# Attention written out step by step, with two score buffers, one bank for turned rows and routing counts, 112-wide two-head tiles, and a shorter last chunk

## The chip, the cores and the metric

The kernel runs on one core of one Trainium2 chip. The metric is device time in microseconds (us) of one launch. Shares of the time are read in one profiled execution. TensorE is PE in the profile (PEld is its weight load), VectorE is DVE, ScalarE is ACT, GpSimd is POOL, and SP is the engine that only issues transfers.

## The reference

A gated linear attention (batch 4, 8 heads, 768 tokens, head size 48) feeds a top-1 mixture of 8 experts, and that feeds a normed gated MLP over 3072 tokens of width 384:

```python
for t in range(S):                       # attention
    state = f[:, :, t, :, None] * state + einsum('bhd,bhe->bhde', k[:, :, t], v[:, :, t])
    y[:, :, t] = einsum('bhd,bhde->bhe', q[:, :, t], state)
logits = x @ w_gate + modality_bias[modality_id]          # experts, x = the 3072 rows of y
e_idx = argmax(logits, axis=1)
h = maximum(x[mask] @ w1[e], 0.0); out[mask] = gate_w[mask, None] * (h @ w2[e])
xn = x / rms * rms_g                                      # MLP
out = (silu(xn @ w_gate) * (xn @ w_val)) @ w_out
```

## The kernel before, in words

The program has two large parts. `attention` takes the first 158 us, `experts` (the experts, then the MLP) the rest. Between them stands a fallback, `general_attention`, which is skipped when a flag is zero; entering and leaving these parts is a barrier of all engines.

In `attention` the 24 tiles of 128 tokens (number n = 4c + b, chunk c = 0 to 5 of the sequence, batch entry b = 0 to 3) pass through a software pipeline. A function `steps` calls one `step(c, b, ...)` for each tile number plus four more (c = 6, called CH), and each engine has its own `step`. `tile(c, b, back)` names the tile that a part of the step works on: the one `back` places behind. The order on each engine is simply the order in which its step is written, and semaphores (`masked`, `x_kept`, `yT_kept` ...) join the engines. Heads go in pairs: one of the two in rows 0 to 47, the other in rows 64 to 111 of the 128 partitions (PAD = 64).

In the step of tile m PE does, in this order: the key turn of tile m-1 (transposes into `ks_ps`, L730), the scores of m-1 (`sc_ps`, L738), the turn-and-gate product of m-3 (`x_ps`, L749, 96 output columns and 8 routing logits per head pair), the state's growth of m-2 (`ds_ps`, L720), and the output of m-2 (`yT_ps`: from the old state L766, from the scores L773). DVE does: scaled keys and queries kT, qT of tile m (L617, L618), the running sum of m+1 (L605), the mask of the scores of m-1 (L627), `grown` of m-2 (L635), and the logits of m-3 read from `x_ps` (L646). ACT does the exponentials, copies `ks`, fades the state (L556), copies `x_group` (L567) and `yT` (L575). POOL clamps the gates of later tiles (L496) and scatters finished rows to the experts' regions in HBM (L137).

Once per chunk the routing is done: `choose` on DVE at b = 2 (L100 to L113), `count` on PE at the end of b = 3 (two small matmuls into `rt_ps`, L117, L118), `place` on DVE at the next b = 0 (L126 to L133). In chunks 3 and 5 a `pick` follows on DVE (L197 to L205): it chooses the expert whose weights SP loads ahead (L208 to L218). In the last four steps ACT and DVE also split these weights into a high and a low part (`hi_w1`, `lo_w1`, L222, L226), and PE turns the first rows of that expert (L233), which SP loads (L218) after the scatters of chunk 3 have landed. The last four scatters stand on POOL behind `place` of chunk 4, and POOL waits for their landing before it leaves the part.

The loop over chunks 2 to 5 is a loop in hardware with two chunks in its body; `ahead` wraps some operations in a branch.

Of the kernel before, what the change touches and what calls it, by code (L numbers as in the profile page):

```python
# [19 lines left out]
PAD = 64  # L20
PR = H // 2
# [223 lines left out]
def attention(nc, qkf, v, w_gate, modality, bias, ident, rt, first, w1, w2, decay, flag, x_regions):  # L245
# [9 lines left out]
    with ExitStack() as ctx:  # L255
# [41 lines left out]
        rt_ps = ps("rt_ps", [P, 3, E])  # L297
        flag_ps = rt_ps[:, 2, 0:1]
# [40 lines left out]
        xT_ps = sc_ps[:].rearrange("p a j t -> p (a j t)")[:, 0:KD * TM].rearrange("p (k t) -> p k t", k=KD)  # L339

        def steps(eng, step):

            for i in range(2 * B):
                step(i // B, i % B, i // B, nullcontext)
            with eng.Fori(1, CH // 2) as i:
                for half in range(2):
                    for b in range(B):  # L350
                        step(i * 2 + half, b, half, (lambda: eng.If(i < CH // 2 - 1)) if half else nullcontext)
            for b in range(B):
                step(CH, b, 0, None)
# [10 lines left out]
        def ahead(b, steps_ahead, more):  # L364
            return more() if b + steps_ahead >= B else nullcontext()

        RT_MADE = 7
        BIAS_STEPS = 4
        PICKS = CH // 2 - 1
# [3 lines left out]

        def x_pairs(s):
            return x_ps[:, s % 2, 0:PR * XG].rearrange("p (j r) -> p j r", j=PR)
# [34 lines left out]
        def _(sp):  # L410
# [48 lines left out]
        def _(pool):  # L459
# [38 lines left out]
            def step(c, b, half, more):  # L498
                if t := tile(c, b, -2):
                    with ahead(b, 2, more):  # L500
                        clamp(t[0], t[1])
# [11 lines left out]
            steps(pool, step)  # L513
# [5 lines left out]
        def _(act):  # L519
# [12 lines left out]
            def step(c, b, half, more):  # L532
# [9 lines left out]
                if (t := tile(c, b, -1)) and not (at(c, 0) and b == 0):  # L542
                    with ahead(b, 1, more):
                        neg_logs(*t)
                if t := tile(c, b, 1):
# [3 lines left out]
                    nc.scalar.copy(ks[:, s], ks_ps[:]).then_inc(ks_done, 1)  # L549
                if (t := tile(c, b, 3)) and not at(c, CH):  # L550
# [7 lines left out]
                    last.then_inc(state_done, 1)  # L558
                if t := tile(c, b, 3):
# [3 lines left out]
                    if not (at(t[0], 0) or at(t[0], 1)):  # L563
# [4 lines left out]
                                   x_pairs(s)[:, :, 0:2 * D]).then_inc(x_copied, 1)  # L568
                if at(c, CH) and b < 2:
                    first.hi_w1(nc, act, 2 * b, ahead_sems)  # L570
                if t := tile(c, b, 2):
                    _, s, n = t
                    act.wait_ge(y_done, n + 1)
                    wait_past(act, x_done, n - 1)
                    nc.scalar.copy(yT[:, s % 2], yT_ps[:]).then_inc(yT_kept, 1)  # L575
                if at(c, CH) and b == 0:
                    first.hi_w1(nc, act, 1, ahead_sems)
                if at(c, CH) and b == 1:
                    first.hi_x(nc, act, xT_ps, ahead_sems)
                if at(c, CH) and b == 2:  # L580
                    first.hi_w1(nc, act, 3, ahead_sems)
# [8 lines left out]
            steps(act, step)  # L590

        @block.vector
        def _(dve):
# [16 lines left out]
            def step(c, b, half, more):  # L610
# [8 lines left out]
                if (t := tile(c, b, -1)) and not (at(c, 0) and b == 0):  # L619
                    with ahead(b, 1, more):  # L620
                        sums(*t)
                if t := tile(c, b, 1):
# [5 lines left out]
                                            sc_ps[:].rearrange("p a j t -> p (a j) t"), keep, ALU.mult).then_inc(masked, 1)  # L628
                if (t := tile(c, b, 2)) and not at(c, CH):
# [8 lines left out]
                if at(c, CH) and b == 2:  # L638
# [4 lines left out]
                if t := tile(c, b, 3):  # L643
                    _, s, n = t
                    dve.wait_ge(x_copied, n + 1)
                    nc.vector.tensor_reduce(rt.logits[:, n, :], x_pairs(s)[:, :, 2 * D:XG].rearrange("p j e -> p e j"),  # L646
# [20 lines left out]
                if at(c, CH) and b == 1:  # L667
                    first.lo_w1(nc, dve, 2, ahead_sems)
                if at(c, CH) and b == 2:
                    first.lo_x(nc, dve, xT_ps, ahead_sems)  # L670
                    first.lo_w1(nc, dve, 3, ahead_sems)
# [33 lines left out]
            steps(dve, step)  # L705

        @block.tensor
        def _(pe):
# [5 lines left out]
            def growth(s, n):  # L714
# [4 lines left out]
                for j in range(PR):  # L719
                    mm = nc.tensor.matmul(ds_ps[:, 2 * D * j:2 * D * (j + 1)], ks[:, s, j],  # L720
# [3 lines left out]
            def step(c, b, half, more):  # L724
                if t := tile(c, b, 1):
                    _, s, n = t
                    pe.wait_ge(scaled, n + 1)
                    wait_past(pe, ks_done, n)
                    for j in range(PR):
                        mm = nc.tensor.transpose(ks_ps[:, j], kT[:, s, j], ident[:])  # L730
# [1232 lines left out]
```

## Time and profile before

| | |
|---|---|
| time, median of 3 runs | 869.16 us (864.9 to 869.27) |
| time of the profiled execution | 866.84 us |
| its span, first to last instruction | 865.1 us |
| PE busy, PEld busy | 833.0 us (96%), 762.5 us (88%) |
| DVE, ACT, POOL busy | 471.8 us (55%), 389.6 us (45%), 165.6 us (19%) |
| mean granted TensorE clock | 0.988 |
| last attention matmul, first matmul of `experts` | 154.20 us, 160.30 us |

The times of the three runs reach over 4.4 us, 0.5% of the time. The 1.7 us between the profiled execution's time and its span lie around the program.

### The profile page before, as it was taken

How to read it: one execution, taken by the hardware profiler on the slowest of the kernel's cores; microseconds unless marked ns; L12 is line 12 of the kernel's file. 1: busy time of each engine (PE TensorE's matmuls, PEld its weight loads, DVE VectorE, ACT ScalarE, POOL GpSimd, SP SyncE). 2: the span in 40 equal slices, each digit the busy share in tenths (PEclk: the TensorE clock that was granted, in tenths of full speed). 3: DMA queues.
4: the chain of work that ended last, by engine and by line, in shares of the span. 5: the costliest groups of instructions: out<-in, count | busy, mean ns of one | idle time of the engine just before them, and what ended most of it. 6: DMA issues, size and time to landing. Idle time of an engine off the chain costs nothing.

```text
span 865.1 us, 15457 instructions
## 1 busy us (share of the span) xinstructions
PE 833.0 (96%) x5332; PEld 762.5 (88%) x5332; DVE 471.8 (55%) x773; ACT 389.6 (45%) x750; POOL 165.6 (19%) x165
## 2 busy tenths in 40 slices
PE   6999999779999999989999999999999999999997
PEld 6798988779999999989888888888888898888887
DVE  7989898687766666653444333334333333433332
ACT  5988786375666555653423411331241133123112
POOL 5444352318554000000000200100020010001001
PEclk9999999889999999999999999999999999999999
DMA  9877666497988797750200200100020000000000
GB/s 182 188 148 169 150 146 210 153 387 239 301 258 260 245 344 255 255 147 20 74 1 1 74 0 1 66 8 0 0 73 0 0 28 8 0 0 36 0 0 36
DMA packets 44082, 96.49 MB, mean 112 GB/s; under 512 B 9168, under 2 KB 25040, under 8 KB 43920
## 3 DMA queue, kind: packets, MB, share of 16 engines
q1 hardware_dynamic: 39952, 85.81, 33.6%
q0 software_dynamic: 3840, 9.47, 3.1%
q10 hardware_dynamic: 256, 0.79, 0.4%
q8 instruction: 18, 0.29, 0.1%
q14 instruction: 16, 0.13, 0.1%
HBM read 76.75 MB, written 19.29 MB: 111 GB/s over the span
## 4 chain that ended last, share of the span: by engine, by line
PE 78%; issue 2%; DVE 1%; POOL 0%; ACT 0%; DVEq 0%; ACTq 0%
PE h_ps L1779 16%; PE h_ps L1781 15%; PE h_ps L1780 15%; PE ym_ps L1779 7%; PE ym_ps L1781 7%; PE ym_ps L1780 7%; PE xTm_ps L1780 3%; PE xTm_ps L1779 3%; PE xTm_ps L1781 3%; PE xT_ps L1796 1%; PE xTm_ps L1787 1%; POOL out L1443 0%; DVE h_lo L1691 0%; DVE w_lo L1664 0%; ACT w_hi L1461 0%
## 5 line engine op out<-in xcount | busy, mean ns | idle before, releaser
L1754 DVE TENSOR_TENSOR gs<-h_ps,sig 128x512 f32<-128x512 f32 x72 | 49.8, 691 | 175.5 <-ACT sig L1555 175.5
L1555 ACT ACTIVATE sig<-h_ps 128x512 f32<-128x512 f32 x72 | 43.1, 598 | 158.9 <-PE h_ps L1781 158.9
L1566 ACT CAST h_hi<-hid 128x512 fp32r<-128x512 f32 x72 | 44.6, 620 | 150.2 <-DVE hid L1757 150.2
L1779 PE MATMUL h_ps<-x_hi,w_hi 128*128 128x256 f32 x312 | 89.7, 287 | 7.7 <-DVEq L1682 5.1
L1781 PE MATMUL h_ps<-x_lo,w_hi 128*128 128x256 f32 x312 | 89.3, 286 | 0.0
L1780 PE MATMUL h_ps<-x_hi,w_lo 128*128 128x256 f32 x312 | 89.1, 285 | 0.0
L1779 PE MATMUL h_ps<-w_hi,wg_hi 128*128 128x512 f32 x216 | 85.5, 396 | 0.0
L1781 PE MATMUL h_ps<-w_lo,wg_hi 128*128 128x512 f32 x216 | 84.6, 392 | 0.0
L1781 PE MATMUL h_ps<-w_lo,wv_hi 128*128 128x512 f32 x216 | 84.2, 390 | 0.0
L1780 PE MATMUL h_ps<-w_hi,wv_lo 128*128 128x512 f32 x216 | 84.0, 389 | 0.0
L1779 PE MATMUL h_ps<-w_hi,wv_hi 128*128 128x512 f32 x216 | 84.0, 389 | 0.0
L1780 PE MATMUL h_ps<-w_hi,wg_lo 128*128 128x512 f32 x216 | 83.9, 388 | 0.0
L1757 DVE TENSOR_TENSOR hid<-h_ps,gs 128x512 f32<-128x512 f32 x72 | 49.8, 692 | 57.5 <-PE h_ps L1781 57.5
L1779 PE MATMUL ym_ps<-w_hi,h_hi 128*128 128x384 f32 x208 | 73.0, 351 | 7.1 <-issue 3.5
L1664 DVE TENSOR_TENSOR w_lo<-w_in,w_hi 128x768 fp32r<-128x768 f32 x52 | 55.1, 1061 | 36.2 <-ACT w_hi L1461 36.1
L1767 DVE TENSOR_TENSOR h_lo<-hid,h_hi 128x512 fp32r<-128x512 f32 x72 | 49.8, 692 | 44.7 <-ACT h_hi L1566 44.7
L1781 PE MATMUL ym_ps<-w_lo,h_hi 128*128 128x384 f32 x208 | 71.2, 342 | 0.0
L1780 PE MATMUL ym_ps<-w_hi,h_lo 128*128 128x384 f32 x208 | 71.0, 342 | 0.0
L1779 PEld LDWEIGHTS h_ps<-x_hi,w_hi 128*128 128x128 f32 x312 | 60.7, 194 | 8.4 <-DVEq L1682 5.2
L1780 PEld LDWEIGHTS h_ps<-x_hi,w_lo 128*128 128x128 f32 x312 | 60.4, 194 | 0.0
L1781 PEld LDWEIGHTS h_ps<-x_lo,w_hi 128*128 128x128 f32 x312 | 60.4, 194 | 0.0
L1461 ACT CAST w_hi<-w_in 128x768 fp32r<-128x768 f32 x52 | 43.3, 835 | 34.2 <-PE ym_ps L1781 27.5
(222 smaller groups left out, 1890.0 us busy)
## 6 DMA issues: line engine op xcount, KB each, us to landing
w_raw<-in_w SPq DMA_DIRECT2D x52, 384.0 KB, 5.0
w_in<-in_w SPq DMA_DIRECT2D x52, 384.0 KB, 5.1
qkf_in<-in_qkf SPq DMA_DIRECT2D x43, 288.0 KB, 5.0
y_sorted<-x_group SPq DMA_DIRECT2D x13, 384.0 KB, 3.4
v_in<-in_v SPq DMA_DIRECT2D x24, 192.0 KB, 4.3
x_regions<-zero_row SPq DMA_DIRECT2D x12, 384.0 KB, 2.9
x_group<-x_regions SPq DMA_DIRECT2D x12, 384.0 KB, 3.9
g_in<-in_wg SPq DMA_DIRECT2D x3, 768.0 KB, 8.1
```

Of the source, the lines that this page charges most:

```text
L1461: nc.scalar.copy(w2_hi[:, 2 * g:2 * g + 2].rearrange("p b d -> p (b d)"), w2_in[:, g]).then_inc(w2_hi_done, 1)
L1555: nc.scalar.activation(sig[:], g_ps, ACT.Sigmoid).then_inc(sig_done, 1)
L1566: nc.scalar.copy(h2_hi[:, fb % HELD], hid[:]).then_inc(h2_hi_done, 1)
L1664: nc.vector.tensor_tensor(w2_lo[:, 2 * g:2 * g + 2].rearrange("p b d -> p (b d)"), w2_in[:, g], w2_hi[:, 2 * g:2 * g + 2].rearrange("p b d ...
L1754: nc.vector.tensor_tensor(gs[:], g_ps, sig[:], ALU.mult).then_inc(gs_done, 1)
L1757: nc.vector.tensor_tensor(hid[:], v_ps, gs[:], ALU.mult).then_inc(hid_done, 1)
L1767: nc.vector.tensor_tensor(h2_lo[:, fb % HELD], hid[:], h2_hi[:, fb % HELD].bitcast(F32), ALU.subtract).then_inc(h2_split, 1)
L1779: nc.tensor.matmul(out, hi, rhs_hi, start=first, stop=False)
L1780: nc.tensor.matmul(out, lo, rhs_hi, start=False, stop=False)
L1781: return nc.tensor.matmul(out, hi, rhs_lo, start=False, stop=last)
L1787: mm = nc.tensor.transpose(xT_ps[:, k, s * P:(s + 1) * P], x_in[:, s, k * P:(k + 1) * P], ident[:])
L1796: mm = nc.tensor.transpose(xT2_ps[:, k % 2, q * P:(q + 1) * P], y_in[par][:, q, k * P:(k + 1) * P], ident[:])
```

## The change

- Order of the loop: `steps` is written out on PE, DVE, ACT and POOL (28 steps, no hardware loop, no branches); SP keeps its loop.
- Buffers: `sc_ps` has two score buffers in place of one, so PE's scores wait for the mask of two tiles before. `x_ps` has one bank in place of two, so PE's turn-and-gate product waits for the logits of the tile before (`x_kept` n in place of n-1). The routing counts live in the same bank, the flag in `ds_ps`.
- The mask wait moves into `read`, ahead of the growth.
- `count` moves from the end of b = 3 to the next b = 0, behind the scores; at b = 1 the product waits until `place` has read the counts.
- Two-head tiles: key turn, ks copy, growth, read of the state and turn-and-gate work on rows (or columns) 0 to 111 in place of 0 to 127 (ROWS = 112).
- For the last four tiles (n >= GROWN = 20) there is no key turn and no ks copy, no growth, no `grown` and no state. Before, growth and `grown` ran for tiles 20 and 21, the key turn for all four, the state for tile 20.
- `pick` runs in chunk 5 alone, and SP issues the eight weight transfers ahead of the last two v transfers.
- Last steps: the x rows ahead are turned right after the output of tile 22, the output of tile 23 goes into `ks_ps`, the products of tiles 22 and 23 stand together at the end, and the last `lo_w1` moves into `experts`, behind `choose`.

```diff
-        sc_ps = ps("sc_ps", [P, 2, PR, P])
+        sc_ps = ps("sc_ps", [P, 2, 2, PR, P])
-        x_ps = ps("x_ps", [P, 2, 512])
+        x_ps = ps("x_ps", [P, 512])
+        rt_ps = x_ps[:, PR * XG:PR * XG + 2 * E].rearrange("p (i e) -> p i e", i=2)
+        flag_ps = ds_ps[:, DM:DM + 1]
-            for i in range(2 * B):
-                step(i // B, i % B, i // B, nullcontext)
-            with eng.Fori(1, CH // 2) as i:
-                for half in range(2):
-                    for b in range(B):
-                        step(i * 2 + half, b, half, (lambda: eng.If(i < CH // 2 - 1)) if half else nullcontext)
+            for c in range(CH):
+                for b in range(B):
+                    step(c, b, c % 2)
...
@@ sync
+            sp.wait_ge(ahead_sems.picked, 1)
+            e = first.expert_of(sp)
+            first.load_weights(sp, e, w1, w2, ahead_sems)
             for b in range(2):
                 load_v(*tile(CH, b, 2))
-            sp.wait_ge(ahead_sems.picked, PICKS)
-            e = first.expert_of(sp)
-            first.load_weights(sp, e, w1, w2, ahead_sems)
@@ vector
-                    if half and not at(c, CH):
-                        first.pick(nc, dve, rt, ahead_sems, (c - 3) * (Ahead.PICKED // 2))
+                    if c == CH - 1:
+                        first.pick(nc, dve, rt, ahead_sems, 0)
@@ tensor
+            def read(c, b, t, acc):
+                cc, s, n = t
+                pe.wait_ge(masked, n + 1)
...
+                if n < GROWN and n > 0:
+                    growth(s, n)
...
-                    wait_past(pe, masked, n)
+                    wait_past(pe, masked, n - 1)
...
-                    wait_past(pe, x_kept, n - 1)
+                    if n < NT - 1:
+                        wait_past(pe, x_kept, n)
+                    if c > 1 and b == 0:
+                        pe.wait_ge(rt_made, RT_MADE)
+                        pe.wait_ge(marks, (c - 2) * Routing.PLACED + Routing.CHOSEN)
+                        rt.count(nc, rt_ps[:, 0], rt_ps[:, 1]).then_inc(counted, 1)
+                    if c > 1 and b == 1:
+                        pe.wait_ge(marks, (c - 2) * Routing.PLACED + Routing.CHOSEN + 2)
...
+                if (t := tile(c, b, 2)) and not (at(c, CH) and b == 1):
+                    read(c, b, t, yT_ps)
+                if at(c, CH) and b == 0:
+                    first.turn(nc, pe, xT_ps, ident, ahead_sems)
@@ experts, vector
             rt.choose(nc, dve, CH - 1, marks, 0)
+            lo_w1(0, GR - 1)
             lo_w2(0, 0)
```

PE at the end of the attention part, from the scores of the last tile (23) on, before. `ident,x_ahead` are the rows turned ahead; `small,ones_r` is the flag:

```order
L738 MATMUL sc_ps<-qT,kT 128x128 [waits masked]
L749 MATMUL x_ps<-turn_gate,yT 128x104 [waits x_kept,yT_kept]
L766 MATMUL yT_ps<-qT,state 128x128 [waits state_done,v_landed2]
L773 MATMUL yT_ps<-scores,v_in 48x128 x8
L749 MATMUL x_ps<-turn_gate,yT 128x104 [waits x_kept,yT_kept]
L766 MATMUL yT_ps<-qT,state 128x128 [waits state_done,v_landed3,masked]
L784 MATMUL rt_ps<-small,ones_r 128x1 [waits small_ready]
L233 MATMUL sc_ps<-ident,x_ahead 128x128 [waits x_ahead]
L749 MATMUL x_ps<-turn_gate,yT 128x104 [waits x_kept,yT_kept]
```

The same place on PE in the changed kernel, in its line numbers:

```order
L752 MATMUL sc_ps<-qT,kT 128x128 [waits masked,scaled]
L118 MATMUL x_ps<-upto,before 128x8 [waits rt_made,marks,x_kept,yT_kept]
L725 MATMUL yT_ps<-qT,state 112x128 [waits state_done,v_landed2,masked]
L234 MATMUL sc_ps<-ident,x_ahead 128x128 [waits x_ahead]
L725 MATMUL ks_ps<-qT,state 112x128 [waits v_landed3,state_done,masked,ks_done]
L759 MATMUL ds_ps<-small,ones_r 128x1 [waits small_ready]
L775 MATMUL x_ps<-turn_gate,yT 128x104 [waits marks,x_kept,yT_kept]
L775 MATMUL yT_ps<-turn_gate,yT 128x104 [waits yT_kept]
```

The key turn ahead of the scores is gone, the counts stand behind the scores, the turn of the rows ahead has moved from behind the last output to ahead of it, and the last two products stand together.

SP behind its loop, before (`expert_ahead` is the number that `pick` leaves; `w_raw` and `w_in` are the weights):

```order
L421 DMA v_in<-in_v 128x384 [waits y_done] x2
L208 TENSOR_LOAD expert_ahead [waits picked]
L212 DMA w_raw<-in_w 128x768
L214 DMA w_in<-in_w 128x768 x4
L218 ISA [waits scattered2,scattered3,scattered1,scattered0]
L218 DMA x_ahead<-x_regions 128x2x384
```

And in the changed kernel:

```order
L209 TENSOR_LOAD expert_ahead [waits picked]
L213 DMA w_raw<-in_w 128x768
L215 DMA w_in<-in_w 128x768 x4
L415 DMA v_in<-in_v 128x384 [waits y_done] x2
L219 ISA [waits scattered2,scattered3,scattered1,scattered0]
L219 DMA x_ahead<-x_regions 128x2x384
```

The eight weight transfers (four rows of `w_raw`, of which one is shown, and four of `w_in`) now stand ahead of v of tiles 22 and 23.

## Rows read from the trace of the kernel before

**Rows 1.** Timeline of PE, counts, back edge, one step: start, length, line, operation

```profile
97.16 0.39 PE L117 MATMUL rt_ps<-upto,before 128*128 128x8 f32 x2
...
97.62 0.63 PE L730 MATMUL ks_ps<-ident,kT 128*128 128x128 f32 x4
...
99.28 1.14 PE L749 MATMUL x_ps<-turn_gate,yT 128*128 128x104 f32 x8
100.25 1.05 PE L720 MATMUL ds_ps<-v_in,ks 128*128 128x96 f32 x8
101.14 1.08 PE L766 MATMUL yT_ps<-qT,state 128*128 128x128 f32 x8
...
103.17 0.66 PE L730 MATMUL ks_ps<-ident,kT 128*128 128x128 f32 x4
103.75 1.16 PE L738 MATMUL sc_ps<-qT,kT 48*128 48x128 f32 x16
```

**Rows 2.** Waits of PE up to 156 us: total, times, longest

```profile
PE sc_ps L738 <- DVE scores L627: 5.4, 6, 1.6
```

**Rows 3.** Timeline of PE behind the pick of chunk 3

```profile
84.99 1.16 PE L738 MATMUL sc_ps<-qT,kT 48*128 48x128 f32 x16 [1.35 <-DVE scores L627]
86.08 1.51 PE L749 MATMUL x_ps<-turn_gate,yT 128*128 128x104 f32 x8
...
90.58 1.08 PE L773 MATMUL yT_ps<-scores,v_in 128*48 128x128 f32 x16
```

**Rows 4.** Busy time by stretch: PE, PEld, DVE, ACT, POOL, then granted clock, DMA share, GB/s

```profile
86.70:90.10 3.40, 3.40 (x18) 3.40 (x18) 3.35 (x6) 1.69 (x6) 2.21 (x2) 0.50 0.97 184
...
160.30:165.10 4.80, 4.80 (x23) 4.80 (x23) 2.31 (x9) 1.42 (x3) 0.48 (x3) 0.50 0.78 253
```

**Rows 5.** Timeline of DVE, first operation of the pick of chunk 3, and after it

```profile
78.87 0.16 DVE L197 TENSOR_TENSOR has<-base,start 128x8 f32<-128x8 f32 x1
...
80.93 1.11 DVE L617 TENSOR_TENSOR kT<-qkf_in,rise 128x512 f32<-128x512 f32 x1
...
85.60 0.19 DVE L646 TENSOR_REDUCE logits<-x_ps 128x32 f32 x1
```

**Rows 6.** Groups of weight loads from 35 to 145 us: busy us, mean ns

```profile
L720 PEld LDWEIGHTS ds_ps<-v_in,ks 128*128 128x128 f32 x152 | 19.4, 199 | 0.0
...
L773 PEld LDWEIGHTS yT_ps<-scores,v_in 128*48 128x48 f32 x304 | 15.7, 123 | 2.3
```

**Rows 7.** Timeline of PE at the end of the attention part

```profile
133.87 1.16 PE L738 MATMUL sc_ps<-qT,kT 48*128 48x128 f32 x16 [1.34 <-DVE scores L627]
134.96 1.14 PE L749 MATMUL x_ps<-turn_gate,yT 128*128 128x104 f32 x8
...
146.53 1.14 PE L749 MATMUL x_ps<-turn_gate,yT 128*128 128x104 f32 x8
160.30 0.55 PE L1779 MATMUL h_ps<-x_hi,w_hi 128*128 128x256 f32 x1 [5.06 <-DVEq L1682]
```

**Rows 8.** Timeline of DVE at the end of the attention part

```profile
134.47 0.19 DVE L646 TENSOR_REDUCE logits<-x_ps 128x32 f32 x1
...
138.17 0.71 DVE L635 TENSOR_TENSOR grown<-ds_ps,state 48x192 f32<-48x192 f32 x2
...
149.28 0.17 DVE L132 CAST row<-row_f 128x4 uint32<-128x4 f32 x1
```

**Rows 9.** Timeline of POOL, first and last of the four last scatters

```profile
150.27 1.30 POOL L137 DMA_INDIRECT x_regions<-x_group,row  x1 [9.38 <-DVE row L132]
...
154.80 0.97 POOL L137 DMA_INDIRECT x_regions<-x_group,row  x1 [0.30 <-issue]
```

**Rows 10.** Timeline of SP's queue: the weights and the rows ahead

```profile
133.79 2.60 SPq L212 DMA_DIRECT2D w_raw<-in_w  x4
...
146.33 0.39 SPq L218 DMA_DIRECT2D x_ahead<-x_regions  x1
```

**Rows 11.** Landing times of x_regions' transfers, 120 to 165 us

```profile
DMA to landing us min/median/max: 2.6/3.0/6.2
```

More of the change, by code:

```diff
@@ L496, in clamp, with step @@
                 nc.gpsimd.tensor_scalar(f, f, LEAST_LOGIT, None, ALU.max).then_inc(clamped, 1)
-            def step(c, b, half, more):
+            def step(c, b, half):
                 if t := tile(c, b, -2):
-                    with ahead(b, 2, more):
-                        clamp(t[0], t[1])
+                    clamp(t[0], t[1])
                 if not (at(c, 0) or at(c, 1)):
@@ L512, in _ @@
             pool.sem_inc(clamped, FIRST_TWO)
-            steps(pool, step)
+            steps(step)
             for b in range(B):
@@ L530, in neg_logs, with step @@
                 nc.scalar.activation(neg_log[:, b % 2, :, 1:P + 1], exp_f[:], ACT.Ln, bias=1.0).then_inc(log_done, 1)
-            def step(c, b, half, more):
+            def step(c, b, half):
                 if t := tile(c, b, 0):
@@ L542, in step @@
                 if (t := tile(c, b, -1)) and not (at(c, 0) and b == 0):
-                    with ahead(b, 1, more):
-                        neg_logs(*t)
-                if t := tile(c, b, 1):
+                    neg_logs(*t)
+                if (t := tile(c, b, 1)) and t[2] < GROWN:
                     _, s, n = t
@@ L558, in step @@
                     last.then_inc(state_done, 1)
+                if at(c, CH) and b == 1:
+                    first.hi_x(nc, act, xT_ps, ahead_sems)
+                    kept(tile(c, b, 2), ks_ps)
+                    first.hi_w1(nc, act, 3, ahead_sems)
                 if t := tile(c, b, 3):
@@ L589, in _ @@
                 neg_logs(0, b, b)
-            steps(act, step)
+            steps(step)
         @block.vector
@@ L608, in sums, with step @@
                                              0.0, ALU.add, ALU.min).then_inc(run_done, 1)
-            def step(c, b, half, more):
+            def step(c, b, half):
                 if t := tile(c, b, 0):
@@ L619, in step @@
                 if (t := tile(c, b, -1)) and not (at(c, 0) and b == 0):
-                    with ahead(b, 1, more):
-                        sums(*t)
+                    sums(*t)
                 if t := tile(c, b, 1):
@@ L637, in step @@
                     last.then_inc(grown_done, 1)
-                if at(c, CH) and b == 2:
+                if at(c, CH) and b == 1:
+                    first.lo_w1(nc, dve, 2, ahead_sems)
+                    first.lo_x(nc, dve, xT_ps, ahead_sems)
                     dve.wait_ge(flag_sum, 1)
@@ L704, in _ @@
             dve.wait_ge(consts, CONSTS)
-            steps(dve, step)
+            steps(step)
         @block.tensor
@@ L777, in step @@
[L777 to L784 removed]
+                if (t := tile(c, b, 2)) and not (at(c, CH) and b == 1):
+                    read(c, b, t, yT_ps)
@@ L785, in step @@
+                if at(c, CH) and b == 0:
                     first.turn(nc, pe, xT_ps, ident, ahead_sems)
-            steps(pe, step)
+            steps(step)
 def general_attention(nc, qkf, v, w_gate, ident, rt, first, w1, w2, x_rows, flag, x_regions):
@@ L1005, in _ @@
                 first.pick(nc, dve, rt, again, 0)
-                for g in range(GR):
+                for g in range(GR - 1):
                     first.lo_w1(nc, dve, g, again)
```

127 lines of the change are left out of this document (55 added, 72 removed).

## The prediction

> **What bounds the kernel now.** The page says that PE is busy almost all the time, so I read its timeline first, then the waits of each engine, then the queues at the end of the attention part, where the next part can only start when all engines have arrived. In a plain step of the attention part PE never idles [rows 1]: the turn-and-gate product takes 100.25 - 99.28 = 0.97 us, the growth 101.14 - 100.25 = 0.89, the output 103.17 - 101.14 = 2.03, the key turn 103.75 - 103.17 = 0.58; the scores take 134.96 - 133.87 = 1.09 [rows 7]. That is 5.56 us for a tile, and all of it is on the path. PE waits for DVE's mask six times, 5.4 us together [rows 2]. So there are three places where the time can change: PE's own work for each tile, these waits, and the end of the part. Behind it, `experts` does the same work as before.
>
> **The wait at the pick of chunk 3, with what it drags along: -3.0 us.** DVE spends 80.93 - 78.87 = 2.06 us on the pick [rows 5], so the mask comes late and PE waits 1.35 us at the scores [rows 3]. The pick of chunk 3 goes. What is late next is the logits read, which now releases the single x bank: it starts at 85.60 [rows 5] and ends 0.19 later, without the pick at 83.7, while PE would reach its product at 84.99 + 1.09 - 1.35 = 84.7. So nothing takes this wait's place: -1.35. Behind the wait the granted clock is 0.50 [rows 4], which is the 1.2 GHz level. From 86.08 to 90.58 PE does the product, the growth and the read of the state [rows 3]: 4.50 us, where a plain step has 103.17 - 99.28 less the other half of the output (1.01), that is 2.88 [rows 1]. The low clock costs 1.6 us here, and it followed directly on that wait. I take it to go with the wait.
>
> **The other waits: -0.5 us, not -2.7.** Two score buffers let PE start the scores without the last mask. But the next thing on PE is the product into the single bank, and it waits for the logits of the tile before, which DVE reads right behind the mask and `grown`. At the pick of chunk 5 one can see both: the scores start at 133.87 and the product at 134.96 [rows 7]; the logits end at 134.47 + 0.19 = 134.66 [rows 8]. With two score buffers and one x bank the product could start at about 134.7 and not at 134.96. So each wait for the mask is not removed but moved one matmul group down and shortened by 0.25 us. Four of the six waits, 5.4 - 1.35 - 1.34 = 2.7 us, are of this kind. I take 0.25 for two of them, since DVE also follows PE and gives only part back; bounds 0 (below that only if the logits come later than now) and 2.7.
>
> **112-wide tiles: -0.9 us.** A weight load of 48 columns takes 123 ns and one of 128 takes 199 [rows 6], 0.95 ns a column, so 16 columns fewer are 15 ns. Eight loads a tile in the growth start 0.111 us apart (0.89/8), and moving 96, 104 or 128 columns nearly the same (0.89, 0.97 and about 1.0 us for eight [rows 1]), so there it is the load that sets the pace: 8 x 14 ns = 0.11 us a tile. The key turn keeps 128-column weights, the read of the state keeps a moving side of 128, so I give them nothing. Twenty tiles would be 2.2 us; but wherever PE then meets DVE's logits (once a chunk, behind `choose`) the last three tiles' gain is lost, since DVE's start did not move as much. I count eight tiles; bounds 0 and 2.2.
>
> **The end of the part: -3.2 us, less 1.7 us of clock.** From the product of tile 19 on PE is free of DVE. Before, that product starts at 134.96, the one of tile 21 at 146.53 [rows 7]. After it starts at 134.7, and up to the end of the product of tile 21 PE has: product 0.97 and output 2.03 of tile 20, scores, product, output (1.09 + 0.97 + 2.03), scores 1.09, counts 0.46 (97.62 - 97.16, [rows 1]), product 0.97. The sum is 9.61, the end 144.3 against 147.5. What is gone is two growths (1.78), two key turns (1.16) and 0.25 of wait. The other two key turns and the growths of tiles before it are gone too, but they lie in the wait for DVE's pick in chunk 5, so PE only waits longer there. DVE keeps up: after 138.17 [rows 8] it has no `grown`, and choose, keys and mask take it to about 142.6, where PE needs tile 20's logits at 143.4. The chain from here to the next part is fixed: logits, `place`, whose rows are written at 149.28 [rows 8], four scatters from 150.27 to 155.8 on POOL, and a landing of 2.6 us more [rows 9, 11], which is 157.4; then the barrier, and PE at 160.30 [rows 7]. DVE's end comes earlier than that: the last `lo_w1` has left, and the last product ends at about 152.5, the logits at 153.3, where POOL comes at 154.2. So the start of `experts` moves with the product of tile 21, by 3.2 us. Against this: PE now idles some 2.7 us around 131 to 134.7 (0.5 for the queries, 2.1 before the product). The wait of 1.35 us at 84.99 had the low clock behind it for 3.4 us [rows 3, 4]; I expect the same here, half of 3.4 us lost: +1.7. Bounds 0 and 1.7.
>
> **What costs nothing.** The weights now stand ahead of v of tiles 22 and 23. Their first transfer now leaves at 133.79 [rows 10], behind the output of tile 19; after it leaves as soon as the pick is done, an estimated 2 us earlier. Eight transfers of 384 KB then stand ahead of v of tile 22, and their issues alone take about 5 us (2.60 for the first four [rows 10]), so v of tile 22 is issued at about 137 and lands, by the longest landing seen [rows 11], at 143; PE wants it at 144.3 or, with the low clock, at 146. If it is late, only the last outputs are late, not `place`; it costs from 0.9 us of lateness on. The rows ahead are turned 7 us earlier in PE's order. They are loaded when the scatter of tile 15 has landed, and a landing takes from 2.6 to 6.2 us [rows 11]; loading starts at 146.33 now [rows 10] and takes 3.0. After, it can be there between 145 and 149, and PE comes at 146.4 (148 with the low clock). The worst is 2.4 us on PE, of which 0.9 is covered by POOL's chain: bounds 0 and +1.5. The moved `lo_w1` (0.95 us) lies in a wait of DVE for ACT's first split in `experts`. The counts keep their four matmuls, behind the scores, where the array would have changed its tiling anyway: 0.
>
> **Hardware loop written out: 0.** The loop's back edge lies between the counts at 97.16 and the key turn at 97.62 [rows 1]: 0.46 us for four matmuls that start 0.11 apart, so there is no pause to remove. The Trainium skill, page Runtime: NRT & Kernel Launch, section Instruction fetch mechanics, says that a taken branch whose target lies outside the stretch of code held breaks the prefetch and costs a fetch, and that straight code therefore pays; by it one back edge would be gained; priced at the shortest landing seen here, 2.6 us [rows 11], the forecast would be 2.6 us lower. The trace shows no such pause at the one back edge that is taken.
>
> **Sum.** -3.0 - 0.5 - 0.9 - 3.2 + 1.7 = -5.9 us against the profiled execution's 866.84: 860.9. The median of the three runs is 2.3 us above that execution, so I put half of it back: 862.0.
>
> **The rivals.**
> *The low clock does not come at the end of the part* (at 133.87 a wait of 1.34 us did not bring it [rows 7]). For it: that row. Against: the idle time is twice as long after. Then -7.6, 860.3. Chance 0.2.
> *The low clock is only moved*, to another place of the attention part or as one stretch more in `experts`, where the start of the part runs at 0.50 for 4.8 us already [rows 4] and its length depends on where the idle time falls. Then -4.2, 863.7. Chance 0.2.
> *The single bank takes it all back*: the x bank binds at every tile, since the logits end only 0.3 us before PE reaches the product in steps with a POOL operation beside DVE. By the rows PE has that slack; if DVE or ACT is 0.4 us later in each of the 12 tiles in which this is close, that is +4.8 and a change of about -1, 867. Chance 0.1.
> *Straight code has to be fetched* (slower). Eight steps more of code stand in the program, on PE some 900 instructions (112 loads and matmuls a step, and the waits), fetched while the tiles' transfers run. If each of the eight steps lost 1.3 us that way, that is 10 us against 5.9: 871. It decides from 0.75 us a step on. Against it: the first eight steps are straight code already and PE has no such stall in them. Chance 0.07.
>
> **How the numbers follow.** Forecast mechanism 0.43, the rivals as above. A measurement of this kernel can tell about 0.5%, 4.3 us. Faster by more than that: the forecast and the first rival, a third of the second, less what of the forecast ends nearer than that: 0.6. Same: 0.32. Slower: 0.08. The range takes the upper bounds of the gains (-3.0 - 1.0 - 2.2 - 3.2, 857.5) and the case of the bank (867.5).
>
> **What the profile after would show.** No wait of over 1 us on PE near 84 us and a clock of 1.00 there; waits on PE at the product L775 and not at the scores L752; the growth at 0.78 us a tile; about 2 us of waiting ahead of the product of tile 19; `experts` starting at 160.30 - 5.9 + 0.2, about 154.5. The prediction is wrong if the scores' waits vanish with nothing at L775, if the growth keeps 0.89, or if the last scatter is not what ends the part.

## The result and the profile after

The changed kernel takes 860.67 us (median of 20 runs, 858.68 to 867.35), the kernel before 868.38 us (20 runs beside it, 863.51 to 870.87). The ratio is 0.9926, 95% interval 0.9913 to 0.994: 0.74% less, 6.4 us by the ratio. Forecast: 862.0, range 857.5 to 867.5.

The page of the profiled execution (859.9 us), engines busy:

```profile
span 858.0 us, 15129 instructions
...
PE 824.7 (96%) x5300; PEld 754.4 (88%) x5300; DVE 465.0 (54%) x760; ACT 385.2 (45%) x742; POOL 169.6 (20%) x165
```

The span is 7.1 us shorter. Where these went can be read by setting the start of the scores (`sc_ps`, which every tile has) of some tiles side by side; the starts are read from PE's timeline of each kernel, the differences are mine:

| stretch | before | after | difference |
|---|---|---|---|
| start to scores of tile 8 | 54.86 | 55.19 | +0.33 |
| tile 8 to tile 12 | 23.14 | 22.40 | -0.74 |
| tile 12 to 16 (the pick of chunk 3) | 25.75 | 22.46 | -3.29 |
| tile 16 to 20 | 23.14 | 22.32 | -0.82 |
| tile 20 to 23 (the pick of chunk 5) | 18.55 | 16.96 | -1.59 |
| tile 23 to the first `h_ps` of `experts` | 14.86 | 15.19 | +0.33 |
| `experts` to the end of the span | 704.80 | 703.48 | -1.32 |

A plain step, timeline of PE after (against [rows 1]):

```profile
54.65 0.60 PE L744 MATMUL ks_ps<-ident,kT 112*128 112x112 f32 x4
55.19 1.16 PE L752 MATMUL sc_ps<-qT,kT 48*128 48x128 f32 x16
56.28 1.14 PE L775 MATMUL x_ps<-turn_gate,yT 112*128 112x104 f32 x8
57.25 0.94 PE L709 MATMUL ds_ps<-v_in,ks 128*112 128x96 f32 x8
58.03 1.05 PE L725 MATMUL yT_ps<-qT,state 112*112 112x128 f32 x8
59.02 1.08 PE L732 MATMUL yT_ps<-scores,v_in 128*48 128x128 f32 x16
```

The growth now takes 58.03 - 57.25 = 0.78 us (0.89 before), the key turn 0.54 (0.58), the read of the state 0.99 (1.02), scores and product as before. Waits of PE, first 156 us (against [rows 2]):

```profile
PE x_ps L775 <- DVE logits L641: 4.1, 3, 2.1
...
PE ks_ps L744 <- DVE qT L612: 3.6, 2, 3.3
```

No wait is left at the scores for a mask; three stand at the single bank instead. Three more (1.8 us in all) stand there under another name: the counts (L118) share the bank and are the first to be held by the tile's logits. The trace puts these waits down to "issue", but the one that ends at 118.21 ends 0.1 us after DVE's logits (117.92 + 0.19).

```profile
72.89 0.36 PE L118 MATMUL x_ps<-upto,before 128*128 128x8 f32 x2 [0.42 <-issue]
```

The place of the pick of chunk 3 (against [rows 3], where these three stood at 86.08, behind it, and 90.58), and the end of the attention part (against [rows 7]):

```profile
84.06 1.14 PE L775 MATMUL x_ps<-turn_gate,yT 112*128 112x104 f32 x8
...
86.80 0.97 PE L732 MATMUL yT_ps<-scores,v_in 128*48 128x128 f32 x14
...
130.74 1.75 PE L775 MATMUL x_ps<-turn_gate,yT 112*128 112x104 f32 x8 [2.08 <-DVE logits L641]
132.28 1.93 PE L725 MATMUL yT_ps<-qT,state 112*112 112x128 f32 x8
134.14 1.20 PE L732 MATMUL yT_ps<-scores,v_in 128*48 128x128 f32 x16
135.28 1.16 PE L752 MATMUL sc_ps<-qT,kT 48*128 48x128 f32 x16
...
140.89 1.12 PE L775 MATMUL x_ps<-turn_gate,yT 112*128 112x104 f32 x8
141.84 1.05 PE L725 MATMUL yT_ps<-qT,state 112*112 112x128 f32 x8
143.83 0.87 PE L234 MATMUL sc_ps<-ident,x_ahead 128*128 128x128 f32 x6
...
154.52 0.55 PE L1776 MATMUL h_ps<-x_hi,w_hi 128*128 128x256 f32 x1 [5.74 <-DVEq L1678]
```

Windows, columns as in [rows 4]; the seventh figure behind the stretch is the granted clock:

```profile
35.50:38.80 3.30, 3.30 (x25) 2.56 (x24) 2.48 (x5) 1.84 (x6) 1.49 (x1) 0.50 0.82 181
84.00:87.40 3.40, 3.40 (x40) 3.21 (x38) 2.99 (x4) 3.37 (x9) 3.19 (x3) 1.00 0.84 167
131.10:134.40 3.30, 3.30 (x19) 3.05 (x20) 3.27 (x6) 1.73 (x6) 1.36 (x1) 0.50 1.03 414
```

The half clock (1.2 GHz) has left the pick of chunk 3. It now follows the new wait of 2.08 us that ends at 130.74, and one stretch more stands early, behind a wait of 1.51 us for the logits that ends at 33.74. Before, a wait of 1.59 us stood at the same place, and no half clock came behind it:

```profile
33.07 1.16 PE L738 MATMUL sc_ps<-qT,kT 48*128 48x128 f32 x16 [1.59 <-DVE scores L627]
...
33.20:40.00 6.80, 6.80 (x78) 6.11 (x79) 5.88 (x12) 5.96 (x16) 2.31 (x2) 1.00 0.90 175
```

POOL at the end (against [rows 9]):

```profile
144.61 1.31 POOL L138 DMA_INDIRECT x_regions<-x_group,row  x1 [8.56 <-DVE row L133]
...
149.22 0.96 POOL L138 DMA_INDIRECT x_regions<-x_group,row  x1 [0.30 <-issue]
154.19 0.14 POOL L1391 IOTA limits<- 128x12 f32 x1 [4.01 <-POOLq L792]
```

The last scatter starts 154.80 - 149.22 = 5.58 us earlier and `experts` 160.30 - 154.52 = 5.78: the scatters' chain still ends the part.

### The profile page after: what moved, and what is told of

Same layout as the page of the kernel before. It is cut to its first block, busy times and chain, and to the rows that moved or that the text cites. A ratio compares the mean times of both kernels' runs of the same rounds, so it can differ in the third digit from the quotient of the medians.

```text
span 858.0 us, 15129 instructions
## 1 busy us (share of the span) xinstructions
PE 824.7 (96%) x5300; PEld 754.4 (88%) x5300; DVE 465.0 (54%) x760; ACT 385.2 (45%) x742; POOL 169.6 (20%) x165
## 4 chain that ended last, share of the span: by engine, by line
PE 77%; DVE 2%; issue 2%; POOL 0%; ACT 0%; DVEq 0%; ACTq 0%
PE h_ps L1776 16%; PE h_ps L1778 16%; PE h_ps L1777 16%; PE ym_ps L1776 7%; PE ym_ps L1778 7%; PE ym_ps L1777 7%; PE xTm_ps L1777 3%; PE xTm_ps L1776 3%; PE xTm_ps L1778 3%; PE xT_ps L1793 1%; PE xTm_ps L1784 1%; POOL out L1439 0%; DVE w_lo L1654 0%; DVE h_lo L1688 0%; DVE w_lo L1660 0%
```

## The experiments

The clock first, since it decides how the profiles can be compared. How much half clock a profiled execution has in its first tiles differs by kernel and run: 3.4 us ahead of the scores of tile 8 before, 6.8 after, up to 17.1 in the runs below. So spans alone mislead. I compare stretches that start at the scores of tile 8, and whole times by their ratio to the kernel before on the same chip.

### The pick and the loop, each alone

The kernel before with the loop written out, and the same with the pick of chunk 5 alone:

```diff
-            for i in range(2 * B):
-                step(i // B, i % B, i // B, nullcontext)
-            with eng.Fori(1, CH // 2) as i:
...
+            for c in range(CH):
+                for b in range(B):
+                    step(c, b, c % 2, nullcontext)
```
```diff
-        PICKS = CH // 2 - 1
+        PICKS = 1
...
-                    if half and not at(c, CH):
+                    if at(c, CH - 1):
```

> Before, with the loop over chunks written out on PE, DVE, ACT and POOL and nothing else changed. My theory: no change, within 0.5 us; the first matmul of the experts part stays within 0.5 us of 160.3 and the wait of 1.35 us near 85 us stays. Rival from the page on instruction fetch: one taken branch less, 2.6 us less. Rival of slow fetching of straight code: pauses on PE that end in issue and not in a semaphore, 6 us more or above.

> Before, with the loop written out and the pick in chunk 5 alone. My theory (the wait behind the pick of chunk 3 brings the low clock with it): against the version that is only written out, the wait of 1.35 us on PE near 85 us and the half-clock stretch behind it are both gone, 3.0 us less, about 0.9965 of the kernel before. Rival (the low clock is not tied to that wait, it comes anyway at another place): 1.4 us less, and one half-clock stretch still stands between 40 and 130 us.

Written out: median 871.07, ratio 1.0017 (0.9993 to 1.0041). One pick: 869.61, ratio 1.001 (0.999 to 1.003). By the times neither is told from no change. The traces say more. From the scores of tile 12 to those of tile 16: 25.75 before, 24.17 written out, 22.70 with one pick. The last step, 1.47 us, is the wait (1.40). The first, 1.58 us, is the clock: with the pick still in place PE waited as before and the half clock did not come. Timeline and window of the written-out kernel:

```profile
89.08 1.16 PE L735 MATMUL sc_ps<-qT,kT 48*128 48x128 f32 x16 [1.40 <-DVE scores L624]
...
89.10:92.50 3.40, 3.40 (x36) 3.28 (x37) 3.32 (x7) 3.35 (x9) 1.60 (x2) 1.00 1.01 202
```

So both sizes of the forecast's first term are right (1.35 and 1.6), but the second is not tied to the wait: it goes with it in some executions.

Otherwise writing the loop out gives and takes. The two mask waits of 0.36 us, at 72.44 and 121.32 before, are gone (four tiles take 22.70 in place of 23.14, twice). From the scores of tile 23 to `h_ps` it takes 15.77 in place of 14.86: ACT begins its last copy of `yT` 0.65 us behind the end of PE's last output (156.01 - 155.36), where it was 0.12 (153.39 - 153.27), and POOL, which waits at the barrier for the others, goes on 6.08 us after its last scatter began (162.97 - 156.89) and not 5.18. Why ACT is late is not shown. Up to `h_ps` these cancel: from the scores of tile 8 it takes 103.95 against 105.44, and the 1.49 us between them are the clock.

Behind that the same kernels show something new. PE, written out, at the start of `experts`:

```profile
163.30 0.55 PE L1776 MATMUL h_ps<-x_hi,w_hi 128*128 128x256 f32 x1 [5.50 <-DVEq L1679]
163.64 0.41 PE L1777 MATMUL h_ps<-x_hi,w_lo 128*128 128x256 f32 x1
163.86 0.41 PE L1778 MATMUL h_ps<-x_lo,w_hi 128*128 128x256 f32 x1
165.43 0.37 PE L1776 MATMUL h_ps<-x_hi,w_hi 128*128 128x256 f32 x1 [1.16 <-issue]
```

Three matmuls, then PE stands for 1.16 us (1.11 with one pick) with nothing to wait for. The kernel before and the changed one have no such stop.

### Where the stop comes from

PE executes 3019 recorded instructions (matmuls, weight loads, waits and the like) ahead of the first matmul of `experts` in both kernels with the stop (their code for PE is the same), 3058 before, 2958 after. The 3058 count the loop's body twice, so they are no place in the code and say little here. Three kernels move this place with idle waits on a mark long given, behind PE's last matmul of the attention part:

```diff
             steps(step)
+            for _ in range(61):
+                pe.wait_ge(small_ready, 1)
```

> The changed kernel with 61 waits on a mark that has long been given behind TensorE's last matmul of the attention part, inside the 5.7 us that TensorE stands there anyway: this moves its instructions of the experts part 61 places on, to where they stand in the two kernels with the loop written out and the old tiles (3019 ahead of the first expert's matmul, against 2958). If the stop of 1.2 us behind the first three matmuls of the experts part in those two hangs on the place of the instructions in the straight code, it comes here as well and the median is about 861.9. If it hangs on something else in those kernels, there is no stop and the median is 860.7. In both cases the wait ahead of the first matmul is a little shorter in the waits and ends at the same place.

> The kernel before with its loop written out, and 64 such waits behind TensorE's last matmul of the attention part. If the stop of 1.2 us hangs on the place of the instructions in straight code, it is gone or stands elsewhere, and the median is 1.2 below that of the written-out kernel, at the kernel before or up to 0.3 above. If it does not, the stop of 1.2 us stays behind the first three matmuls and the median is that of the written-out kernel, 1.5 above the kernel before.

> Two waits are taken up by one instruction, so the 61 waits of the run before moved TensorE's instructions 31 places and not 61 (2989 ahead of the first expert's matmul, 3019 in the kernels with the stop). This kernel is the changed one with 122 waits: 61 places. If the stop hangs on the place alone, it stands behind the first three matmuls of the experts part, 1.1 to 1.2 us long, and the median is about 861.9. If there is no stop, something besides the place is needed for it, and the median is that of the changed kernel, 860.7.

| kernel | instructions ahead | stop | ratio |
|---|---|---|---|
| changed | 2958 | none | 0.9926 (0.9913 to 0.994) |
| changed, 61 waits | 2989 | none | 0.9939 (0.9918 to 0.9959) |
| changed, `GROWN` at 22 (below) | 3006 | none | 0.9961 (0.9938 to 0.9983) |
| changed, 122 waits | 3020 | 1.43 us | 0.9977 (0.9954 to 1.0001) |
| written out | 3019 | 1.16 us | 1.0017 (0.9993 to 1.0041) |
| written out, 64 waits | 3052 | none | 1.0006 (0.9982 to 1.0031) |

The first expectation rested on one instruction for each wait, and two share one (61 waits add 31 instructions), so the first kernel did not reach the place. The one with 122 waits did, and the stop came back in a kernel that had none. PE there:

```profile
161.48 0.55 PE L1778 MATMUL h_ps<-x_hi,w_hi 128*128 128x256 f32 x1 [7.96 <-DVEq L1680]
161.83 0.41 PE L1779 MATMUL h_ps<-x_hi,w_lo 128*128 128x256 f32 x1
162.04 0.41 PE L1780 MATMUL h_ps<-x_lo,w_hi 128*128 128x256 f32 x1
163.89 0.58 PE L1778 MATMUL h_ps<-x_hi,w_hi 128*128 128x256 f32 x1 [1.43 <-issue]
```

The place in the instruction stream decides, for these places. That the stop is a fetch of instructions is a reading and is not shown: a 16 KB instruction packet (queue q8) starts 0.18 us ahead of the first matmul written out and 0.20 us ahead of it in the changed kernel, which has no stop. The Trainium skill, page Runtime: NRT & Kernel Launch, section Instruction fetch mechanics, says that each engine fetches its next block of code while it executes the current one, and that a taken branch can break this. The trace shows the stop behind such a branch: PE jumps over `general_attention` at 161.99 (COMPARE_BRANCH, L851, written out), 1.3 us ahead of the first matmul. Every kernel here takes that branch, with the stop or without, so these runs don't tell whether the stop belongs to straight code or to the code behind a branch.

The median with 122 waits missed its expectation (866.88 against 861.9), for another reason: 122 waits keep PE from the barrier for too long. From PE's last product to `h_ps` it is 161.48 - 152.46 = 9.02 us, against 154.52 - 147.72 = 6.80 after. These 2.2 and the 1.4 of the stop are 3.6 of the 4.4 us by which its ratio is above that of the changed kernel; that the half clock had 10.6 us from the scores of tile 8 to `experts` and 13.3 behind, against 6.4 and 7.2, is of a size for the rest.

### 112 or 128 wide

```diff
-ROWS = PAD + D
+ROWS = P
```

> After, with the two-head tiles 128 wide again (ROWS = 128). In the profile of after the key turn takes 0.53 us, the growth 0.78 and the read of the state 0.98, where before it was 0.58, 0.89 and 1.02, so 0.20 us a tile. My theory: PE meets DVE's logits once a chunk, so only part of 20 x 0.20 = 4 us comes back: the experts part starts 1.5 us later (1 to 2), and the waits for the logits in chunks 2 to 5 shrink. Rival (all of it is on the path): 4 us later, 1.005 of after. Rival (none is): no change.

Median 864.40, ratio 0.9948 (0.9927 to 0.9969), against 0.9926: 1.9 us more, with intervals that touch. Timeline of PE in this kernel:

```profile
60.87 1.14 PE L775 MATMUL x_ps<-turn_gate,yT 128*128 128x104 f32 x8
61.84 1.05 PE L709 MATMUL ds_ps<-v_in,ks 128*128 128x96 f32 x8
62.73 1.08 PE L725 MATMUL yT_ps<-qT,state 128*128 128x128 f32 x8
63.74 1.08 PE L732 MATMUL yT_ps<-scores,v_in 128*48 128x128 f32 x16
64.75 0.66 PE L744 MATMUL ks_ps<-ident,kT 128*128 128x128 f32 x4
65.34 0.93 PE L752 MATMUL sc_ps<-qT,kT 48*128 48x128 f32 x11
```

From scores to scores it is 65.34 - 59.77 = 5.57 us a tile, against 60.56 - 55.19 = 5.37. But from the scores of tile 8 to `experts` it is 100.07 against 99.33, only 0.7 us for 12 such tiles (2.4). The rest lies in the waits at the counts, 0.42, 0.47 and 0.88 us after, which this kernel hasn't: there DVE sets the pace of the chunk, and what PE saves it waits. The expectation, 1.5 us (1 to 2), lies between the two readings, and neither decides it.

### One score buffer

```diff
-                    wait_past(pe, masked, n - 1)
+                    wait_past(pe, masked, n)
```

> After, where PE's scores wait for the mask of the tile before again, as with one score buffer (the banks stay as they are). My theory: with a single x bank the scores and the product behind them are held by DVE's mask and logits, which end about 1 us apart, so the second score buffer hides little: up to 0.25 us in each of the six places where PE waits, 0.5 us at the start of the experts part, and no change in time that can be measured. Rival (the second buffer is what removed the waits): 2.5 us more or above, 1.003 of after.

Median 865.07, ratio 0.9948 (0.9927 to 0.9969). PE's waits here:

```profile
PE sc_ps L752 <- DVE scores L620: 8.3, 8, 2.4
```

Eight waits of 8.3 us in place of 4.1 + 1.8 at the bank (L775 and L118). From the scores of tile 8 to `experts` it takes 100.38, 1.05 us more than after. So the second buffer moved the waits to the bank and took a part off them, as expected, but a larger one: 1.05 us by the trace and 1.9 by the ratios, with intervals that overlap, where 0.5 was expected.

### The last tiles' growth

```diff
-        GROWN = NT - B
+        GROWN = NT - 2
```

> After, with GROWN = 22 in place of 20: tiles 20 and 21 get their key turn, ks copy, growth, grown and state back; the output does not change. My theory: the two growths (2 x 0.78) lie behind the product of tile 19, where PE is the limit, the two key turns lie in PE's wait for DVE's logits; the experts part starts 1.6 us later. Rival (both on the path): 2.6 us later. Rival (DVE is the limit at the end of the part): its two grown operations count, 1.5 us, and PE waits at the product of tile 20 or 21. If the PE wait before the product of tile 19 shrinks below 1.3 us, the half-clock stretch there may go too and take back 1.6 us.

Median 865.63, ratio 0.9961 (0.9938 to 0.9983). PE at the product of tile 19:

```profile
131.97 1.11 PE L775 MATMUL x_ps<-turn_gate,yT 112*128 112x104 f32 x8 [1.54 <-DVE logits L641]
132.91 0.94 PE L709 MATMUL ds_ps<-v_in,ks 128*112 128x96 f32 x8
```

From there to the end of the product of tile 21 it is 143.04 - 131.97 = 11.07 us, and 141.84 - 130.74 = 11.10 after. The two growths (1.56) are hidden by the absence of the half clock, which costs the changed kernel 0.57 + 0.88 + 0.13 = 1.58 in this stretch (product, read of the state and output of 1.54, 1.86 and 1.14 us against 0.97, 0.98 and 1.01). In this kernel it fell elsewhere, to 96.5, behind a wait of 0.88 us at the counts, and four tiles take 24.50 there in place of 22.46. From the scores of tile 8 to `experts` it is 100.81 against 99.33, 1.5 us more, where 1.6 was expected; the ratios differ by 3.0 us, with intervals that touch.

### Transfers and landings at the end

The v transfers ahead of the weights again; and the landing of the last four scatters waited for in `experts`, by those who need the rows, and not by POOL at the end of the attention part:

```diff
+            for b in range(2):
+                load_v(*tile(CH, b, 2))
             sp.wait_ge(ahead_sems.picked, 1)
...
-            for b in range(2):
-                load_v(*tile(CH, b, 2))
```
```diff
-            pool.wait_ge(ended, 16 * B)
...
+                    sp.wait_ge(first.ended, 16 * B)
                     sp.wait_ge(scattered, 16 * B)
                     load_x(1)
```

> After, with SP's last two v transfers ahead of the weights again, as before. My theory: nothing hangs on it, since the rows ahead are turned (143.83 us) without a wait and the outputs of tiles 22 and 23 wait for no v: 0, within 0.3 us at the start of the experts part. Rival (the earlier weights are what let the rows ahead land in time): PE waits for x_ahead or ACT for the weights, 1 to 2.4 us later.

> After, where the landing of the last four scatters is waited for in the experts part (by POOL behind its own four scatters, by SP ahead of loading the rows of tile 1, by ACT ahead of the copy of the first rows) and no longer at the end of the attention part. My theory: POOL's chain from place over four scatters to their landing sets the start of the experts part; without the landing POOL ends its part at about 150.2 us in place of 151.8 and the part starts 1.6 us sooner (1 to 2), and what comes sooner is kept to the end. Rival (DVE or ACT is the last at the barrier, or the first tile of the experts part waits for the landing): less than 0.5 us.

v first: median 862.76, ratio 0.9935 (0.9912 to 0.9958), not told from the changed kernel by the times. But the trace shows the expectation's rival and not its theory. SP stands at the v transfers, which wait for outputs, so the weights leave at 134.73 and not at 127.43, the rows ahead at 146.91 and not at 140.61, and PE waits for them:

```profile
149.82 1.41 PE L234 MATMUL sc_ps<-ident,x_ahead 128*128 128x128 f32 x6 [3.28 <-DMA x_ahead<-x_regions]
...
151.67 0.97 POOL L138 DMA_INDIRECT x_regions<-x_group,row  x1 [0.30 <-issue]
159.40 0.14 POOL L1391 IOTA limits<- 128x12 f32 x1 [6.76 <-POOLq L792]
```

The last scatter no longer ends the part: from it to POOL's next work it is 7.73 us in place of 4.97. From the end of the product of tile 21 to `h_ps` it takes 159.72 - 144.48 = 15.24, against 12.68 after, 2.6 us more. In this execution most of it was won back ahead of that: the wait in front of the product of tile 19 was 1.13, and no half clock came behind it. It stood at 122.7 instead, behind a wait of 0.88 us.

Landing later: median 859.51, ratio 0.9899 (0.9877 to 0.9922), 2.3 us below the changed kernel, with intervals that overlap a little. POOL:

```profile
154.75 0.96 POOL L138 DMA_INDIRECT x_regions<-x_group,row  x1 [0.30 <-issue]
157.32 0.14 POOL L1393 IOTA limits<- 128x12 f32 x1 [1.60 <-POOLq L792]
```

2.57 us from the last scatter to POOL's next work, where it was 154.19 - 149.22 = 4.97. From the scores of tile 23 to `h_ps` it is 12.79 in place of 15.19, all of the 2.4 us; 1.6 (1 to 2) was expected. So the landing did end the part. This execution has a stretch of half clock behind a wait of 0.89 us at the counts, which ends at 75.60:

```profile
76.70:80.00 3.30, 3.30 (x19) 3.30 (x18) 3.23 (x6) 1.41 (x5) 0.00 (x0) 0.50 0.75 165
```

### The logits read ahead of `grown`, and both edits

```diff
+                if (t := tile(c, b, 3)) and not at(c, CH):
+                    keep_logits(t[2])
                 if (t := tile(c, b, 2)) and t[2] < GROWN:
...
-                if t := tile(c, b, 3):
-                    _, s, n = t
-                    dve.wait_ge(x_copied, n + 1)
...
```

> After, with DVE's read of the logits (0.19 us) ahead of grown (0.71 us) in each step. The single x bank is then free 0.7 us sooner behind the mask. My theory: PE's waits in front of the counts and the product (0.42, 0.47, 0.88, 0.49, 1.51 and 2.08 us in the profile of after) shrink by up to 0.7 us each; the experts part starts 1 to 2.5 us sooner, more if a half-clock stretch goes with them. Rival (ACT's copy of x and not DVE's order holds the logits): DVE waits for x_copied ahead of the logits, grown comes later, and the part gets no shorter or some tenths longer.

Median 858.72, ratio 0.9892 (0.9868 to 0.9915). The wait ahead of the product of tile 19 is 1.31 in place of 2.08, but PE now waits 0.75 in place of 0.21 for the queries at the scores in front of it, so little is won there. Those at the counts of two chunks are gone: four tiles take 21.94 us (from tile 8 to 12 and from 12 to 16), which is 4 x 5.37 and the counts' 0.46, in place of 22.40 and 22.46. There the bank was the last thing that held PE.

```profile
129.69 1.70 PE L779 MATMUL x_ps<-turn_gate,yT 112*128 112x104 f32 x8 [1.31 <-DVE logits L663]
```

> The changed kernel with both edits that came out below it: VectorE's first-expert logits are read ahead of the grown rows, and the landing of the last four scatters is waited for in the experts part. If the two save in different places (the one in the step of the last groups, the other at the start of the experts part), the sum is about 860.7 - 2.0 - 1.2 = 857.5. If the two only moved stretches of half granted clock about, it is no lower than the better of the two, 858.7 or more.

Median 858.13 of 4 runs (857.5 expected), ratio 0.9859 (0.9831 to 0.9886): 1.4% below the kernel before and below the changed kernel, whose interval starts at 0.9913. Each edit alone is not clear of the changed kernel (0.9915 and 0.9922 are their upper ends), and the two together are not clear of each alone. The ratios of the two edits, taken from that of the changed kernel, add up to 0.9926 - 0.0034 - 0.0027 = 0.9865. `experts` starts at 152.42, and from the scores of tile 8 it takes 96.59 us, against 97.62 with the first edit alone and 99.33 after.

## Why the prediction was right, and where only its sum was

**The pick of chunk 3: right.** Forecast -3.0. Between tiles 12 and 16 it was -3.29. With 0.8 for four narrower tiles and +0.47 for the new wait at the counts, 2.96 are left for the pick. The written-out kernel shows that "I take it to go with the wait" does not hold: the wait was there and the half clock was not. That its 1.6 us came out is in part luck.

**The other waits: wrong sign.** Forecast -0.5. Ahead of the product of tile 19, without both picks, the waits were 5.4 - 1.35 - 1.34 = 2.7 us and are 0.49 + 0.26 + 1.51 + 0.42 + 0.47 + 0.88 = 4.0: +1.3. "Moved one matmul group down" was right; "shortened" was not. Tiles that became shorter bring PE to the bank earlier, while DVE comes when it came. The one early wait of 1.51 had a stretch of half clock behind it, which I had only as a rival; before, the wait of 1.59 at this place had none.

**112-wide tiles: mis-sized twice.** The growth was right to the hundredth (0.78). "The key turn keeps 128-column weights ... so I give them nothing" failed: it now turns 112 columns, 0.54 against 0.58, and the read of the state takes 0.99 against 1.02. It is 0.20 a tile, not 0.11. And it comes at about 20 tiles, 4 us gross, of which the waits above take back a large part. The forecast's net of 0.9 stands beside 0.7 from tile 8 on by the trace and 1.9 by the ratios.

**The end of the part: right.** -3.2 + 1.7. From the product of tile 19 to the end of that of tile 21 it is 11.10 us; the forecast's 9.61 + 1.7 is 11.31. The half clock came, for 1.58. Behind it the chain of logits, rows, scatters and landing is the same to 0.12 us (12.80 before, 12.68 after). PE waited 0.21 + 2.08 there (2.7 forecast). That the half clock came was more likely than not by the runs, and no more: with 1.54 (`GROWN` at 22) and 1.13 (v first) at this place it did not. `experts` starts at 154.52; the text said about 154.5.

**Costs of nothing.** Weights ahead of v, and the rows ahead turned earlier: no matmul of the changed kernel waits at either, but the rows are only just in time. They are loaded at 140.61, take 3.1 us to land, and the weight load that turns them at 143.8 waits 0.2 for them. With the logits first PE waits 0.72 there, with `GROWN` at 22 0.96, and POOL's chain covers both; with v first it is 3.28 and costs 2.6. So this order of the transfers is not free to choose, as "nothing hangs on it" had it. The written-out loop: 0 was right for this kernel, by its place in the code. Nothing in the rows of before could show it. In the two kernels that differ from before by little else, 0.9 us of waits are won and 0.9 lost up to `h_ps`, and a stop of 1.1 to 1.2 us follows. The rival *Straight code has to be fetched* asked for a loss in each step and had none; what exists is one stop at one place.

**The rivals.** *The low clock is only moved* was half true: one stretch came at 35.4 within the attention part, and one fewer is in `experts`, where the time behind `h_ps` fell by 1.3 us. This is not an effect of the change that I could show: among the profiled executions without the stop that time goes with the stretches of half clock in it (698.93 us of matmuls with 7.0 us of it, one score buffer; 700.92 with 13.7, both edits), whatever the attention part does. That is why the profiled span fell by 7.1, where the attention part gave 5.8 (5.9 forecast). *The single bank takes it all back* had the right mechanism and a quarter of its size.

Summed as measured up to the product of tile 19: pick -2.96, other waits +1.3, early half clock +1.6, narrower tiles about -3.8, the wait at the pick of chunk 5 from 1.34 to 2.29, +0.95, less the two key turns in front of it, -1.16: -4.07, where the trace has 130.74 - 134.96 = -4.22. Two errors of 1.8 and 1.6 us on one side and one of 2.9 on the other cancelled in the sum. So the 5.8 us were hit by luck as much as by the mechanism: the pick and the end of the part were right, the terms between them were not.

Open: how much of the second score buffer and of the 112-wide tiles is in the times. Both are 1.9 us by the ratios, with intervals of about 0.2% each way.

## What to carry to other kernels

When two buffers become one and one becomes two, follow the order of the engine that releases them: here DVE's read of the logits stood behind `grown`, which nobody on PE needed so soon, and setting it ahead gave 0.34% more by the ratios, 1.7 us by the trace from tile 8 on. A saving on the waited-for engine is lost wherever the other engine sets the pace of the loop, so count it per tile gross and then take off the waits it creates. At the end of a part ask for each wait ahead of the barrier whether the next part's first work needs it; the landing of four scatters did not, and moving its wait gave 0.27% by the ratios, 2.4 us by the trace.

## What the hardware showed that I had not expected

- The length of a wait does not decide whether the half clock follows. Behind waits of 1.3 to 1.6 us it did at 84.99 before (1.35), with the logits first at 129.69 (1.31) and at 33.74 after (1.51); it did not at 33.07 before (1.59), at 133.87 before (1.34), at 89.08 written out (1.40) and at 131.97 with `GROWN` at 22 (1.54). At the pick of chunk 5 the same code waited the same 1.40 us written out, without it, and with 64 idle waits behind, with it. It even followed waits of 0.88 or 0.89 us in four kernels (`GROWN` at 22, v first, landing later, and the logits first at 34.33), while the same wait at 118.21 after had none. Behind the waits of 2.07 to 2.38 us ahead of the product of tile 19 or the scores in front of it, it came in all six kernels that have one (changed, 128 wide, one score buffer, 61 and 122 waits, landing later).
- A stop of 1.1 to 1.4 us without any wait, behind three matmuls of a new part, that comes and goes with the number of instructions ahead of it (at 3019 and 3020, not at 2958, 2989, 3006 and 3052), 1.3 us behind a branch that all kernels take.
- Idle waits behind an engine's last work are free only up to a number: 61 moved nothing, 122 delayed the barrier by 2.2 us.
- Single profiled executions differ by up to 13.7 us in how long the half clock lasts ahead of tile 8 (3.4 to 17.1), and by 6.4 us in when they get to that tile (54.86 before to 61.30 written out with 64 waits).
